# Attention in 24 unrolled steps, with q and k turned earlier, row sums from the weighing product and the gate summed token by token

## The reference

```python
# attention: batch 2, heads 8, 768 positions, head size 64, all float32
k_sum = k.reshape(B, H, nb, block, D).max(axis=3)       # blocks of 32: 24 of them
v_sum = v.reshape(B, H, nb, block, D).mean(axis=3)
scores_l = scale * np.matmul(q, k.transpose(0, 1, 3, 2))
mask_l = np.abs(pos[:, None] - pos[None, :]) < window   # window 16
scores_s = scale * np.einsum('bhsd,bhnd->bhsn', q, k_sum) + np.log(block)
scores_all = np.concatenate([np.where(mask_l, scores_l, -1e9), scores_s], axis=-1)
a = np.exp(scores_all - np.max(scores_all, axis=-1, keepdims=True))
a = a / (np.sum(a, axis=-1, keepdims=True) + 1e-09)
attn_out = np.matmul(a, np.concatenate([v, v_sum], axis=2))
# tokens (1536 x 512) -> gate and noise logits (8 + 8 columns) -> the best two of
# eight experts for each token -> their two layers (512 x 1024, ReLU, 1024 x 512),
# weighted and added -> a last dense pair (512 x 2048, leaky ReLU, 2048 x 512)
```

## Time and profile before

| | us |
|---|---|
| median of 3 runs | 862.5 (859.2 to 863.46) |
| the profiled execution, time | 858.7 |
| its span, first to last instruction | 857.1 |
| its first score product | 14.2 |
| its first score product of pairs 1, 2, 3, 4, 5, 6, 7 | 33.2, 47.8, 63.4, 82.5, 100.4, 119.2, 133.9 |
| its last sum of gate logits ends, and the routing starts | 159.9 |
| its first expert product | 189.0 |

### The profile page before, as it was taken

The page is one execution under the profiler, slowest core; times in us unless marked ns, Lnnn a source line. Parts: engine busy times, 40 slices in busy tenths (PEclk is TensorE's granted clock), DMA queues, the critical chain, the costliest instruction groups (busy, mean ns, idle before and its releaser), DMA issues.

```text
span 857.1 us, 12330 instructions
## 1 busy us (share of the span) xinstructions
PE 776.6 (91%) x3850; PEld 646.8 (75%) x3851; DVE 308.9 (36%) x562; ACT 232.4 (27%) x524; POOL 379.1 (44%) x335
## 2 busy tenths in 40 slices
PE   3777798349999999999999999989999999999997
PEld 2766677147888888888888888868878887888886
DVE  6686657542122212212221222134444324432223
ACT  2464546202121212121212121223322222222221
POOL 4687700037568696888788978331011000000000
PEclk9887789759999999999999999999999999999999
DMA  8989864028962637444435353316111100000001
GB/s 214 253 182 271 155 105 68 19 79 258 325 246 86 212 119 256 148 137 145 161 120 172 110 184 98 93 55 201 46 50 42 57 1 24 24 24 24 0 1 50
DMA packets 87389, 103.13 MB, mean 120 GB/s; under 512 B 55648, under 2 KB 61792, under 8 KB 86944
## 3 DMA queue, kind: packets, MB, share of 16 engines
q0 software_dynamic: 17008, 59.52, 21.3%
q1 hardware_dynamic: 69296, 43.22, 19.7%
q10 hardware_dynamic: 1056, 0.03, 0.1%
HBM read 80.89 MB, written 23.69 MB: 122 GB/s over the span
## 4 chain that ended last, share of the span: by engine, by line
PE 75%; DVE 8%; DMA 6%; POOL 4%; issue 3%; ACT 2%; SPq 1%; DVEq 0%; POOLq 0%; ACTq 0%
PE p L1203 33%; PE p L1287 5%; PE p L1289 5%; PE p L1288 5%; PE p L1302 5%; PE p L1304 5%; PE p L1303 5%; DMA x_by_tile<-x_ring 3%; PE p L1195 3%; PE p L1068 2%; PE p L1091 2%; PE p L1108 2%; POOL x_ring L514 2%; PE p L1190 1%; POOL w_lo L475 1%
## 5 line engine op out<-in xcount | busy, mean ns | idle before, releaser
L475 POOL TENSOR_TENSOR w_lo<-stage,w_hi 128x1024 fp32r<-128x1024 f32 x72 | 171.7, 2385 | 6.0
L1203 PE MATMUL p<-w_hi,xT_hi 128*128 x248 | 100.1, 404 | 2.6 <-DVE xT_lo L934 1.9
L1203 PE MATMUL p<-w_hi,xT_lo 128*128 x248 | 97.4, 393 | 0.0
L1203 PE MATMUL p<-w_lo,xT_hi 128*128 x248 | 97.4, 393 | 0.0
L1203 PE MATMUL p<-w_hi,hT_hi 128*128 x240 | 96.5, 402 | 0.0
L1203 PE MATMUL p<-w_lo,hT_hi 128*128 x240 | 93.9, 391 | 0.0
L1203 PE MATMUL p<-w_hi,hT_lo 128*128 x240 | 93.5, 390 | 0.0
L560 POOL DMA_INDIRECT y_pick<-y_by_tile,slots x20 | 19.1, 955 | 166.2 <-PE p L1274 149.7
L473 POOL TENSOR_SCALAR w_hi<-stage 128x1024 fp32r<-128x1024 f32 x72 | 75.9, 1054 | 20.2 <-DMA stage<-in_moe_w 16.5
L1287 PE MATMUL p<-f_xT_hi,w_hi 128*128 (+2 forms) x200 | 77.8, 389 | 1.7 <-DVE f_xT_lo L983 1.7
L934 DVE TENSOR_TENSOR xT_lo<-p,xT_hi 128x512 fp32r<-128x512 f32 x31 | 21.4, 692 | 154.5 <-ACT xT_hi L666 154.5
(11 more groups left out here) (189 smaller groups left out, 1343.6 us busy)
## 6 DMA issues: line engine op xcount, KB each, us to landing
stage<-in_moe_w POOLq DMA_DIRECT2D x64, 512.0 KB, 5.1
y_by_tile<-y_row SPq DMA_DIRECT2D x31, 256.0 KB, 2.0
x_by_tile<-x_ring POOLq DMA_DIRECT2D x28, 256.0 KB, 4.7
x_row<-x_by_tile SPq DMA_DIRECT2D x28, 256.0 KB, 3.0
qk_nat<-in_q SPq DMA_DIRECT2D x16, 192.0 KB, 3.6
qk_nat<-in_k SPq DMA_DIRECT2D x16, 192.0 KB, 4.0
stage<-in_v SPq DMA_DIRECT2D x3, 1024.0 KB, 6.0
v_win<-in_v SPq DMA_DIRECT2D x8, 384.0 KB
```

What stands on the lines that cost most here:

```text
L475: pool.tensor_tensor(w_lo[:, par, cols], stage[:, c % STAGES, :], w_hi[:, par, cols].bitcast(F32), ALU.subtract).then_inc(lo_split, 1)
L1203: last = nc.tensor.matmul(bank, a, w, start=(c == 0 and i == 0), stop=(c == left_hi.shape[1] - 1 and i == 2))
```

## The change

- **Order.** 24 steps, all unrolled, no loop. In step c PE does `score(c)`, `turn_probs(c-1)`, one of `turn_k(n+1)`, `gate_turn(n-2)` and `turn_q(n+2)`, and `weigh(c-2)`. So q is turned nearly two pairs ahead of its use and k one pair less a step. SP, ACT and DVE follow the same order, and SP loads q and k apart.
- **k.** The turned q and k lie in `p01` from column 128 on, with 16 columns of zeros on either side, and one ACT copy of 96 columns for each unit, overlapping in the source, takes the place of the three (`k_part`). The copy of the maxima into `kT` moves from DVE to ACT (`k_means`).
- **Sums.** `v_win` has 65 columns for each unit, the last of ones, so `weigh` gives the row sum as a 65th column. The exponentials no longer give sums.
- **Weighing.** One product for each unit and head, 64 x 65: 8 in a step in place of 4 of 128 x 128. Two units share the 128 partitions of the output, so DVE normalises a step by one multiplication of 128 partitions, and adds eps reading from PSUM.
- **The gate.** `x_out` holds 128 tokens in a row, so `gate_turn` is 6 transposes, and `gate_multiply` is 6 products with the turned tokens stationary and 16 gate columns moving, behind a `weigh`, into a free part of its bank. The copy of the logits and their transposes back fall away, and one DVE addition takes them.
- **Means of v.** From DVE to POOL, as halving additions: for each of three loads, additions of 1024, 512, 256, 128 and 64 columns and a scaling. They stand ahead of POOL's weight pieces. The zeros of `q_diag` move from POOL to DVE.

```diff
-            v_win = sb("v_win", [KC, 2, 2, UNITS, D], where=room)
+            v_win = sb("v_win", [KC, 2, 2, UNITS, VC], where=room)
...
-            x_out = sb("x_out", [P, GROUPS, GU, 2 * D], where=room)
+            x_out = sb("x_out", [P, 2, GROUPS, GU // 2, 2 * D], where=room)
...
+        turned = p01[:, AT:AT + S]
+        k_windows = bass.AP(p01, AT - WINDOW, [list(p01[:].ap[0]), [QB, UNITS], [1, WK]])
...
+            def block_means(i):
+                rows = stage[:, 2 * (i % 2):2 * (i % 2) + 2, :].rearrange("p a n -> p (a n)")
+                pool.wait_ge(v_nat_loaded[i], 16)
+                half = BLOCK * D // 2
+                while half >= D:
+                    link(pool.tensor_tensor(rows[:, 0:half], rows[:, 0:half], rows[:, half:2 * half], ALU.add))
+                    half //= 2
+                pool.tensor_scalar(v_mean[:, i, :], rows[:, 0:D], 1.0 / BLOCK, 1.0, ALU.mult, ALU.mult).then_inc(v_mean_done, 1)
...
-                    last = nc.scalar.activation(probs[:, b, u, :], scores[:, b, u, :], ACT.Exp, bias=negmax[:, b, u:u + 1],
-                                                accum_out=sums[:, s, g, u:u + 1])
+                    last = nc.scalar.activation(probs[:, b, u, :], scores[:, b, u, :], ACT.Exp, bias=negmax[:, b, u:u + 1])
...
-                nc.scalar.copy(kT[:, s, :, WINDOW:WINDOW + QB], units).then_inc(own_k_ready, 1)
-
-                nc.scalar.copy(kT[:, s, 1:, 0:WINDOW], units[:, 0:UNITS - 1, QB - WINDOW:])
-                nc.scalar.copy(kT[:, s, 0:UNITS - 1, WINDOW + QB:WK], units[:, 1:, 0:WINDOW]).then_inc(k_ready, 1)
+                nc.scalar.copy(kT[:, n % 2, :, 0:WK], k_windows).then_inc(k_ready, 1)
...
-                nc.vector.tensor_scalar_add(sums[:, s, g], sums[:, s, g], EPS).then_inc(eps_added, 1)
...
-                for h in range(2):
-                    rows = slice(h * QB, (h + 1) * QB)
-                    last = nc.vector.tensor_tensor(x_out[0:QB, g, :, h * D:(h + 1) * D], o_bank[b][rows, :, h * D:(h + 1) * D],
-                                                   recip[rows, s, g].unsqueeze(2).to_broadcast([QB, GU, D]), ALU.mult)
...
+                nc.vector.tensor_scalar_add(totals[:, b], o_bank[b][:, :, D], EPS).then_inc(eps_added, 1)
...
+                nc.vector.tensor_tensor(x_out[:, n % 2, g].rearrange("p u (h d) -> p (u h) d", h=2), o_bank[b][:, :, 0:D],
+                                        recip[:, b].unsqueeze(2).to_broadcast([P, GU, D]), ALU.mult).then_inc(x_ready, 1)
...
-                    last = nc.tensor.matmul(o_bank[b][:, u, :], probsT[:, b, u * P:(u + 1) * P], v_win[:, s, :, g * GU + u, :], start=True, stop=True)
+                    for h in range(2):
+                        to = o_bank[b][(u % 2) * QB:(u % 2 + 1) * QB, u // 2 * 2 + h, :]
+                        last = nc.tensor.matmul(to, probsT[:, b, u * P + h * QB:u * P + (h + 1) * QB], v_win[:, n % 2, h, g * GU + u, :], start=True, stop=True)
...
+                for j in range(first, end):
+                    last = nc.tensor.matmul(bank[:, j * 2 * E:(j + 1) * 2 * E], xT_gate[:, j * P:(j + 1) * P], gate_w[:, m % (H // 2), :], start=True, stop=True)
```

More of the change, by code:

```diff
@@ L36 @@
 KC = WK + NB
-GR = 256
+VC = D + 1
+AT = P
 MASKED = -1e9
@@ L55 @@
 ROWS = 2
-GP = S // GR
-GM = GP * 2 * E
+GM = TPB * 2 * E
 STAGES = 4
@@ new lines, in _ @@
+            q_part(0)
+            k_blocks(0)
+            q_part(1)
+            dve.wait_ge(consts_done, 3)
+            for n in range(PAIRS):
+                for g in range(GROUPS):
+                    c = GROUPS * n + g
+                    if c >= 3:
+                        normalise(c - 3)
+                    softmax_max(c)
+                    if g == 1 and n + 1 < PAIRS:
+                        k_blocks(n + 1)
+                    if g == 2 and n + 2 < PAIRS:
+                        q_part(n + 2)
@@ L831, in _ @@
+            for c in range(STEPS - 3, STEPS):
+                normalise(c)
+            dve.wait_ge(gate_multiplied, PAIRS)
+            add_logits(PAIRS - 1, last_gate_bank)
             row = lambda i: r_sc[:, i, :]
@@ L1141, in _, with gate_turn @@
-            pe.wait_ge(consts_done, 2)
+                m = gate_beside(c)
+                if m is not None:
+                    gate_multiply(m, gate_bank[b])
+            def gate_turn(m, first=0, end=TPB):
+                pe.wait_ge(x_ready, GROUPS * m + (end + 1) // 2)
+                pe.wait_ge(k_ready, min(m + 4, PAIRS))
+                if m >= 1 and first == 0:
+                    pe.wait_ge(gate_xT_ready, m)
+                for j in range(first, end):
+                    last = nc.tensor.transpose(turned[:, j * P:(j + 1) * P], x_out[:, m % 2, j // 2, j % 2, :], ident[:])
+                last.then_inc(gate_turned, 1)
@@ new lines, in gate_multiply @@
+            def gate_multiply(m, bank, first=0, end=TPB):
+                if m == 0:
+                    pe.wait_ge(small_loaded, 32)
+                pe.wait_ge(gate_xT_ready, m + 1 + (first > 0))
+                for j in range(first, end):
+                    last = nc.tensor.matmul(bank[:, j * 2 * E:(j + 1) * 2 * E], xT_gate[:, j * P:(j + 1) * P], gate_w[:, m % (H // 2), :], start=True, stop=True)
+                if end == TPB:
+                    last.then_inc(gate_multiplied, 1)
+            pe.wait_ge(consts_done, 1)
@@ L1142, in _ @@
+            pe.wait_ge(zeros_done, 1)
             turn_q(0)
             turn_k(0)
[L1144 to L1154 removed]
```

529 lines of the change are left out of this document (238 added, 291 removed).

## The result

| | before | after |
|---|---|---|
| median of the runs | 862.98 (859.2 to 865.9) | 833.5 (829.91 to 840.09) |
| the profiled execution | 858.7 | 829.91 |
| its span | 857.1 | 828.3 |
| gate logits complete | 159.8 | 130.2 |
| first expert product | 189.1 | 159.3 |

The ratio is 0.967, with a 95% interval of 0.9598 to 0.9741: some 29 us faster. The time lies in the range that the prediction gave, 807 to 840, and 15.5 us above its forecast of 818. All of the gain is in the attention, 29.7 us by the logits (before, 159.51 + 0.33 of the earlier trace rows); the rest moved as one block, to within 1 us. The profiled execution of after is the fastest of its four, which lie between 829.9 and 840.1, so a single profile places the logits only to some us.

A forecast was written before the change was run, and what follows sets the result against it. It took PE's gaps and low clock in the attention as the bound: logits at 34.5 + 5 x 12.3 + 11.8 + 7.8 = 115.6 against 159.9, 44.3 us less, so 814.4 profiled and 818 us median; range 807 to 840.

The follow-up runs named there:

- e8: The kernel before, with all 16 of POOL's weight pieces put behind the attention: 898.3 us in one time, gate logits complete at 147.4 us.
- e1: The kernel after, with POOL's 16 weight pieces put behind the last step of the attention: 864.4 us in one time, gate logits complete at 114.1 us.
- e7: The kernel after, with q and k turned where before had them and all 16 weight pieces behind the attention: 882.2 us in one time, logits at 130.4.

## What to carry to other kernels

When a change makes every engine's work shorter, ask next what the same bytes need in the shorter time: here a stage of 130 us holds 124 us of packet time of all 16 DMA engines, PE waited where the share stood at 1.16, and two other orders of the loads brought nothing, while taking 16 weight pieces away brought 16 us. Look also for holes in the share, as the one of 0.22 ahead of the crowd. Cost a transfer from the moment at which its queue reaches it, not from the moment at which its data is ready. Idle time of an engine is no free room: eight of POOL's pieces, moved out of the attention, gave back 10.5 us there and cost 14 in the routing, since DVE waits for them.

## What the runs showed of the hardware

- A DVE instruction that reads and writes SBUF, beside a POOL addition of 128 x 1024, ends when POOL's ends: 2.39 us for 96 columns that take 0.26 alone. One that reads PSUM beside the same addition took 0.25. The eps addition agrees: reading SBUF it took 576 ns in before and 164 in e8, without the pieces; reading PSUM it took 159 in after and in e1.
- A DMA issue is not of fixed length: the halo load (L294) of pair 2 held SP for 0.84 us in e1 and for 5.84 in after, beside POOL's weight loads, with the engines at a share of 1.08 and 371 GB/s in that time. Without pieces it can be long too: 3.70 us in the start of e1.
- Products with 64 columns loaded and 65 moving cost 0.041 us a piece, under the 0.078 of the 64-column transposes of before, which load 128. The weight loads stand for 0.17 us ahead of such a group.
- Fully fed, PE keeps the clock at 1.00 through five pairs (e1). Of six gaps of 2.06 us in e7, one was followed at once by a score of 2.03 us, another by one of 1.28, and four by warm ones.
